# A skipped turn ahead of TensorE's loop, logits two tiles back, and other orders of group work and loads

## The reference

```python
ret = (scale * q @ k.T * Dmat) @ v          # per batch and head; Dmat: causal powers of gamma
x = ret of all heads side by side            # 4608 x 512
logits = x @ phi                             # 4608 x 32
d = softmax of logits over tokens;  c = softmax of logits over slots
slot_in = d.T @ x                            # 32 x 512
slot_out = relu(slot_in[e] @ w1[e]) @ w2[e]  # expert by expert, 4 slots each
y = c @ slot_out
out = ((y @ f1) * (y @ f2)) @ w3 @ w_out     # 4608 x 512
```

## Time and profile before

| | |
|---|---|
| time, median of 3 runs | 393.9 us (393.32 to 394.62) |
| profiled execution, its own time | 393.96 us |
| its span | 392.2 us |
| TensorE busy | 354.2 us (90% of the span) |
| DVE, ACT, POOL busy | 165.3, 125.7, 161.8 us |
[...]
| moved by DMA | 104.77 MB, mean 267 GB/s |

### The profile page before, as it was taken

How to read it: one execution, slowest core, us unless ns; L and a number is a source line. 1 busy time by engine, 2 the same in 40 slices (tenths; PEclk the granted TensorE clock), 3 DMA queues, 4 the chain that set the end, 5 groups by cost and what they waited for, 6 DMA issues and landing times. The chain is left out here.

```text
span 392.2 us, 16043 instructions
## 1 busy us (share of the span) xinstructions
PE 354.2 (90%) x7123; PEld 272.9 (70%) x7123; DVE 165.3 (42%) x329; ACT 125.7 (32%) x276; POOL 161.8 (41%) x155
## 2 busy tenths in 40 slices
PE   1557787899999999899999999899999999999996
PEld 1446676778878878664656555478878888888885
DVE  0333444557657656573013000699853323233320
ACT  1001112322423332222324220532734444434442
POOL 1621222323334542033546451298955554554530
PEclk9988989999999999999999999999999999999999
DMA  7995999768878887879999996058226655556322
GB/s 246 422 370 208 391 427 427 282 241 300 300 246 297 311 308 229 306 288 418 424 428 424 427 425 277 3 90 236 75 92 235 225 188 191 191 176 234 116 107 107
DMA packets 25914, 104.77 MB, mean 267 GB/s; under 512 B 2660, under 2 KB 5284, under 8 KB 16164
## 3 DMA queue, kind: packets, MB, share of 16 engines
q1 hardware_dynamic: 25892, 104.47, 71.2%
HBM read 94.14 MB, written 10.32 MB: 266 GB/s over the span
## 5 line engine op out<-in xcount | busy, mean ns | idle before, releaser
L558 POOL TENSOR_TENSOR pkg_sb<-pkg_sb,const_sb 128x512 f32<-128x512 f32 x36 | 37.5, 1042 | 106.9 <-DMA pkg_sb<-in_tiles 106.9
L620 POOL TENSOR_TENSOR feat<-c_sb 128x512 f32<-128x512 f32 x45 | 56.8, 1273 | 46.2 <-PE psum L988 44.3
L988 PE MATMUL psum<-m_hi,feat_hi 128*128 128x512 f32 x144 | 56.1, 390 | 0.3 <-DVE m_lo L1474 0.3
L988 PE MATMUL psum<-m_lo,feat_hi 128*128 128x512 f32 x144 | 56.0, 389 | 0.0
L988 PE MATMUL psum<-m_hi,feat_lo 128*128 128x512 f32 x144 | 56.0, 389 | 0.0
L427 DVE TENSOR_TENSOR feat_lo<-feat,feat_hi 128x512 fp32r<-128x512 f32 x34 | 27.2, 799 | 62.2 <-ACT feat_hi L1144 61.0
L1004 ACT COPY x_nat<-psum 128x512 f32<-128x512 f32 x36 | 21.1, 585 | 84.0 <-PE psum L700 84.0
L645 PE MATMUL psum<-pkg_sb 64*64 64x64 f32 x1152 | 26.4, 229 | 22.8 <-POOL pkg_sb L558 16.4
L1244 DVE TENSOR_TENSOR x_t<-psum,x_decay 128x512 f32<-128x512 f32 x36 | 24.9, 691 | 47.9 <-PE psum L690 47.9
L1144 ACT CAST feat_hi<-feat 128x512 fp32r<-128x512 f32 x45 | 28.1, 626 | 39.1 <-POOL feat L620 39.1
L690 PE MATMUL psum<-weights_t,pkg_sb 64*64 64x64 f32 x1152 | 32.4, 227 | 7.0 <-issue 4.9
(11 more groups left out here) (138 smaller groups left out, 569.3 us busy)
## 6 DMA issues: line engine op xcount, KB each, us to landing
pkg_sb<-in_tiles SPq DMA_DIRECT2D x34, 1024.0 KB, 4.8
unit_a<-in_units SPq DMA_DIRECT2D x16, 1024.0 KB, 14.5
c_sb<-c_rows SPq DMA_DIRECT2D x45, 256.0 KB
unit_x<-in_units SPq DMA_DIRECT2D x9, 1024.0 KB, 14.1
out<-out_sb SPq DMA_DIRECT2D x36, 256.0 KB, 2.0
fold_raw<-in_fold SPq DMA_DIRECT2D x6, 1024.0 KB, 11.6
unit_y<-in_units SPq DMA_DIRECT2D x5, 1024.0 KB, 12.2
unit_n<-in_units SPq DMA_DIRECT2D x4, 1024.0 KB, 11.6
```

What stands on the lines that cost most here:

```text
L558: nc.gpsimd.tensor_tensor(v_nat(n).rearrange("p (h d) -> p h d", h=HEADS), v_nat(n).rearrange("p (h d) -> p h d", h=HEADS), decay.unsqueez ...
L620: nc.gpsimd.tensor_tensor(feat[:, k, :], c_sb[:, s, x, :], c_sb[:, s, y, :], ALU.mult).then_inc(feat_ready, 1)
L988: last = mm(psum[:, OUT + b, :], x, y, start=(at == 0 and m == 0), stop=(at == 4 and m == 2))
```

## The change

TensorE's loop gets a tenth turn in front, i = 0. In it, each of the four steps is stepped over by a branch, and the scores and update of tile 0 (`first_steps`) run at the end of this turn, behind the steps in the code. In every other turn each step stands behind the same test, and the number of the turn in all other tests is one higher. Within a step, the order becomes: scores and update of the next tile, dispatch (one tile later than before), logits of the tile *two* before, the wait for `x_t` of the tile before, `through_states`, the wait for the copy of the logits, phase 0, `turn_x` of the tile before, phase 1. ACT copies logits before x accordingly and does group work one tile later; DVE does each part of the group work one tile later and ahead of `scale_x`. SP loads the constants first, and of the first two tiles the second half (k and v) ahead of the first (q and k turned); one unit follows tile 3 instead of two, two follow tile 4, two tile 5, one tile 8; the raw weights follow tiles 10, 11, 14 and 15. Behind the loop, the last logits stand ahead of the last `turn_x`.

The diff, cut to what the argument speaks of:

```diff
--- before.py
+++ after.py
@@ -53,6 +53,7 @@
 NAT_RING = 12
 QUARTERS = 4
 EARLY = 3
+FOLD_AT = (10, 11, 14, 15)
 FOLD_HI_AT, FOLD_LO_AT = (18, 22, 26), (21, 23, 25, 27, 29, 31)
 
 
@@ -458,11 +459,10 @@
                 sp.dma_start(pkg_sb[:, t, lo:hi], pkg[t].rearrange("(p c) -> p c", p=P)[:, lo:hi]
                              ).then_inc(tile_loaded[t] if half else first_loaded[t], 16)
 
-            load_first(0, 0)
             sp.dma_start(const_sb[:, 0:C_LATE], consts[:, 0:C_LATE]).then_inc(const_loaded, 16)
-            load_first(0, 1)
-            load_first(1, 0)
-            load_first(1, 1)
+            for t in range(2):
+                load_first(t, 1)
+                load_first(t, 0)
             sp.dma_start(x_decay[:, :, 0:P], consts[:, C_XDECAY:C_ALL].rearrange("p (a n) -> p a n", a=PAIRS)
                          ).then_inc(decay_loaded, 16)
             sp.dma_start(const_sb[:, C_LATE:C_XDECAY], consts[:, C_LATE:C_XDECAY]).then_inc(const_late_loaded, 16)
@@ -470,13 +470,16 @@
             load_tile(2)
             load_tile(3)
             load_first_unit(0)
-            load_first_unit(1)
             for n in range(SLOTS_IN, NTILES):
                 load_tile(n)
-                if n < 2 * SLOTS_IN:
-                    load_first_unit(n - 2)
-                elif n < 3 * SLOTS_IN:
-                    load_fold(n // 2 % 2 * 2, n % 2)
+                if n < SLOTS_IN + 2:
+                    load_first_unit(2 * n - 7)
+                    load_first_unit(2 * n - 6)
+                elif n == 8:
+                    load_first_unit(5)
+                elif n in FOLD_AT:
+                    at = FOLD_AT.index(n)
+                    load_fold(at // 2 * 2, at % 2)
 
             def load_unit(u):
 
...
@@ -694,12 +697,12 @@
                             last.then_inc(phase_done if phase == 0 else out_ready, 1)
                         elif phase == 1:
                             last.then_inc(phase_done, -1)
+                        elif half == 0:
+                            last.then_inc(x_t_ready if a == 0 else logits_copied, -1)
 
             def turn_x(r):
                 for a in range(PAIRS):
                     last = nc.tensor.transpose(psum[:, X_NAT, P * a:P * (a + 1)], x_t[:, r % 2, a, :], ident)
-                    if a < 2:
-                        last.then_inc(x_t_ready if a == 0 else logits_copied, -1)
                 last.then_inc(x_turned, 1)
 
             def logits(r):
@@ -714,7 +717,7 @@
             def dispatch(g):
 
                 pe.wait_ge(exp_nat_ready, g + 1)
-                pe.wait_ge(x_nat_ready, NTILES if g == GROUPS - 1 else dispatched_at(g))
+                pe.wait_ge(x_nat_ready, NTILES if g == GROUPS - 1 else dispatched_at(g) - 1)
                 def nat(t):
                     return x_nat[:, (g * TILES + t) % NAT_RING, :]
 
@@ -735,48 +738,51 @@
                 scores(r)
                 update(r)
 
-            def turn(r):
-
-                pe.wait_ge(logits_copied, 1)
-                pe.wait_ge(x_t_ready, 1)
-                turn_x(r)
-
             def step(i, r):
-                before, after = (r + SLOTS_IN - 1) % SLOTS_IN, (r + 1) % SLOTS_IN
+                two_before, before, after = [(r + m) % SLOTS_IN for m in (SLOTS_IN - 2, SLOTS_IN - 1, 1)]
 
                 if r < SLOTS_IN - 1:
                     next_scores(after)
                 else:
-                    with pe.If(i < NTILES // SLOTS_IN - 1):
+                    with pe.If(i < NTILES // SLOTS_IN):
                         next_scores(after)
-                if r > 0:
-                    turn(before)
+                for g in range(GROUPS - 1):
+                    if dispatched_at(g) % SLOTS_IN == r:
+                        with pe.If(i == dispatched_at(g) // SLOTS_IN + 1):
+                            dispatch(g)
+                if r > 1:
+                    logits(two_before)
                 else:
-                    with pe.If(i > 0):
-                        turn(before)
+                    with pe.If(i > 1):
+                        logits(two_before)
+
+                pe.wait_ge(x_t_ready, 1)
                 through_states(r)
+                pe.wait_ge(logits_copied, 1)
                 through_scores(r, 0)
                 if r > 0:
-                    logits(before)
+                    turn_x(before)
                 else:
-                    with pe.If(i > 0):
-                        logits(before)
-                for g in range(GROUPS - 1):
-                    if dispatched_at(g) % SLOTS_IN == r:
-                        with pe.If(i == dispatched_at(g) // SLOTS_IN):
-                            dispatch(g)
-
+                    with pe.If(i > 1):
+                        turn_x(before)
                 pe.wait_ge(phase_done, QUARTERS)
                 through_scores(r, 1)
 
-            pe.wait_ge(first_loaded[0], 16)
-            pe.wait_ge(v_ready, 1)
-            scores(0)
-            update(0)
-            pe.wait_ge(states_ready, 1)
-            with pe.Fori(0, NTILES // SLOTS_IN) as i:
+            def first_steps():
+
+                pe.wait_ge(first_loaded[0], 16)
+                pe.wait_ge(v_ready, 1)
+                scores(0)
+                update(0)
+                pe.wait_ge(first_loaded[1], 16)
+                pe.wait_ge(states_ready, 1)
+
+            with pe.Fori(0, NTILES // SLOTS_IN + 1) as i:
                 for r in range(SLOTS_IN):
-                    step(i, r)
+                    with pe.If(i > 0):
+                        step(i, r)
+                with pe.If(i == 0):
+                    first_steps()
 
             def fold_part(n):
 
@@ -852,9 +858,12 @@
                     if n is not None:
                         fold_part(n)
 
+            logits(SLOTS_IN - 2)
             fold(1)
-            turn(SLOTS_IN - 1)
+            pe.wait_ge(logits_copied, 1)
+            pe.wait_ge(x_t_ready, 1)
             logits(SLOTS_IN - 1)
+            turn_x(SLOTS_IN - 1)
             fold(5)
 
             dispatch(GROUPS - 1)
...
@@ -1080,27 +1090,28 @@
-            act.sem_inc(logits_copied, 1)
+            act.sem_inc(logits_copied, 2)
...
+                if g > 0 and n == dispatched_at(g - 1):
+                    copy_sums(g - 1)
+                if n > 1:
+                    copy_logits(n - 2)
+                copy_x(n - 1)
+                if g > 0 and t == 1:
                     move_parts(g - 1)
...
@@ -1300,6 +1311,7 @@
                 tt(c_nat[:, g * TILES:(g + 1) * TILES, :], comb[:, :, :],
                    comb_red[:, 3, 0:TILES].unsqueeze(2).to_broadcast([P, TILES, SLOTS]), ALU.mult).then_inc(c_ready, 1)
 
+            dve.sem_inc(x_t_ready, 1)
             dve.wait_ge(const_loaded, 16)
             nc.vector.memset(state_sb[:, 0, :, :].rearrange("p a n -> p (a n)"), 0.0)
             mask_scores(0)
@@ -1314,12 +1326,12 @@
                 else:
 
                     dve.sem_inc(states_ready, 1)
-                scale_x(n)
                 if g > 0:
-                    for at, part in ((0, max_parts), (1, max_slots), (2, turn_exp), (3, turn_raw), (4, max_combine),
-                                     (5, shift_combine), (6, sum_combine), (7, divide_combine)):
+                    for at, part in ((1, max_parts), (2, max_slots), (3, turn_exp), (4, turn_raw), (5, max_combine),
+                                     (6, shift_combine), (7, sum_combine), (8, divide_combine)):
                         if t == at:
                             part(g - 1)
+                scale_x(n)
 
             def w_low(half):
                 for f in range(4):
```

More of the change, by code:

```diff
@@ L380, in dispatched_at @@
         def dispatched_at(g):
-            return g * TILES + TILES + 3
+            return g * TILES + TILES + 4
         def chunks(engine, step):
@@ L490, in _ @@
                 if u == 9:
-                    sp.wait_ge(logits_ready, SUBS * NTILES)
+                    sp.wait_ge(x_turned, NTILES)
                 if u == 11:
@@ L1012, in copy_logits @@
                     act.wait_ge(exp_ready, g - 1)
-                copy(logits_raw[:, g % 2, SLOTS * t:SLOTS * (t + 1)], psum[:, RAW, 0:SLOTS]).then_inc(logits_copied, 1)
-                if t == TILES - 1:
+                copy(logits_raw[:, g % 2, SLOTS * t:SLOTS * (t + 1)], psum[:, RAW, 0:SLOTS]
+                     ).then_inc(group_copied if n == NTILES - 1 else logits_copied, 1)
+                if t == TILES - 1 and n < NTILES - 1:
                     copy(mark[:, :], const_sb[0:1, 0:1]).then_inc(group_copied, 1)
@@ L1081, in relu_hidden @@
                                          ACT.Relu).then_inc(hid_ready, 1)
-            act.sem_inc(logits_copied, 1)
-            for n in range(NTILES):
+            act.sem_inc(logits_copied, 2)
+            for n in range(1, NTILES):
                 g, t = divmod(n, TILES)
-                if n > 0:
-                    copy_x(n - 1)
-                    if g > 0 and n == dispatched_at(g - 1):
```

(14 more changed lines are left out.)

## The result

The changed kernel takes 399.28 us (median of 4 runs, 398.44 to 401.85) against 394.12 us: 1.4% slower, ratio 1.014 (95% interval 1.0102 to 1.0177). The forecast was 387.8 us, 382.0 to 392.5. The profiled execution took 399.35 us, its span is 397.6 us.

A forecast was written before the change was run, and what follows sets the result against it. Bytes were taken to bound the tile stage from 37 to 74 us, TensorE from then on. The sum was 394.0 - 22.2 + S + 1.5 = 373.3 + S, so 387.8 us with S = 14.5; range 382.0 to 392.5.

The forecast's parts named there:

- The start, S: Start of tile 0's scores, behind three code fetches in a row: 14.5 us, bounds 10.9 to 18.7; before 8.77.
- The hidden fetches: Rival for the turn in front: blocks arrive before transfers fill up, S 7.8 us, time 381.1 us; chance 0.13.
- TensorE starts too late: Rival: a fourth fetch or longer ones; S 19.8 or 24.6, time 393.1 or 397.9 us, slower; chance 0.09.
- 373.3: Forecast total in us without the start: 394.0 - 22.2 + 1.5; S is added to it.
- From S to tile 12: Bytes moved in SP's new order: tile 12 in at S + 49.1, its scores at S + 50.3, gain 22.2 - S.
- The hole: Idle transfers in the tile stage: earlier holes before 37 us close, a new one runs from some 18 us to S + 9.2.
- The bytes moved behind tile 12: Two of four raw blocks leave the queue ahead of tile 12: 4.9 us; sharing with tiles 14 and 15 costs at most 0.5.
- the full part: Tile stage from 37 to 74 us, taken as bound by bytes: DMA engines 0.98 busy at 401 GB/s.
- the stretch that has room: Where the two raw blocks go, behind tile 12; from 74 us TensorE was taken as the bound.
- The later turns: Loop turns of four tiles, 13.89 us before: +0.14 a turn; +1.5 us for all later effects, bounds -1 and +5.
- The new wait: Phase 0 waits for the logits' copy, ready at 0.91 us, TensorE there at 0.85: 0.06 a step, 0.24 a turn.
- the old three: Three dispatch tests a turn, ahead of phase 1 before: hidden behind the update, saving 0.42 us a turn.

The follow-up runs named there:

- experiment 6: Changed kernel with two branches in the turn in front, each over two steps, instead of four over one each: 400.71 us, ratio 1.0173.
- experiment 5: Changed kernel with SP holding the loads of tiles 2 and 3 and the unit behind them until tile 0's scores are done: 398.73 us, ratio 1.0136.
- experiment 15: Kernel before, with TensorE waiting ahead of tile 0's scores until tile 3 has landed, nothing else: 398.87 us, ratio 1.0115.
- Experiment 9: Changed kernel, turn in front kept, with all six first units behind tile 3: 393.96 us, ratio 1.0004.
- 10: Changed kernel without the turn in front, with all six first units behind tile 3: 394.76 us, ratio 1.0044.
- experiment 1: Changed kernel without the turn in front, all its other edits kept: 393.01 us, ratio 0.9992.
- experiment 3: Changed kernel with the units and raw weights placed as in the kernel before: 398.11 us, ratio 1.0108.
- 11: Changed kernel without the turn in front and with units and raw weights placed as in the kernel before: 393.38 us, ratio 0.9996.
- 13: Changed kernel without the turn; two units behind tile 3, raw weights quartered behind tiles 4 to 20, other units behind 15, 24, 33, 34: 390.28 us, ratio 0.9894.
- 14: Changed kernel with the turn; two units behind tile 3, raw weights quartered behind tiles 4 to 20, other units behind 15, 24, 33, 34: 392.98 us, ratio 0.9981.
- experiment 4: Kernel before with the new order of units and raw weights alone: 393.12 us, ratio 0.9993.
- experiment 2: Kernel before with the turn in front alone: 400.98 us, ratio 1.0194.

## Why the prediction was wrong

**The start, S: mis-sized.** The mechanism was there, and so were its parts: three jumps, one behind the other, the code behind them loaded and kept, no stall afterwards. In after the branches over the four steps (L782) begin at 1.0, 1.4, 6.7 and 12.1 us and last 0.36, 5.17, 5.35 and 7.25 us, and the q8 row counts one block from 19 to 30 us and none from 30 to 165. That this row is TensorE's code shows in the kernel before: its blocks begin to move at 16.1, 20.6, 26.4, 31.6 and 34.7 us (windows of 0.1 us), and TensorE resumes 2.2 to 2.7 us behind each (18.56, 22.80, 28.65, 34.06 and 37.38). Between two resumptions the trace has 204 to 233 matmuls and weight loads; the rest of the about 256 instructions, waits, branches and skipped code, is my count.

The size was off. I took 3.3 us for the first fetch and 4.7 for the others, S = 14.5, with 18.7 as the most I allowed. No run shows 3.3, 4.7 or 5.9 us as the time of a fetch: they are times between two resumptions, and that a fetch takes as long was my estimate. The runs show in their place what a jump took. Tile 0 started at 19.64: 6.2 us a jump over the 18.6 us from the first branch at 1.0 us. Two jumps took 11.9 us (experiment 6), 6.0 each, and three with the bulk loads held back 18.3 (experiment 5), 6.1 each. Five blocks were fetched by 19 us for three jumps, so two that nobody needed yet were in the row. Why a jump takes longer than the time between two resumptions, no run shows.

What I named as the reason for a long fetch, full transfers, holds in part. Where they ran out, a block moved 2.6 us (experiment 5) and 2.7 us (experiment 15) sooner behind the event before it. But experiment 5 took only 0.4 us off the start, so it is not what made S 5.1 us too small. The hidden fetches (0.13) are refuted: the third block moved at 9.6 us, beside full transfers (0.99 busy from 4.2 to 9.6 us).

The rival that came true is *TensorE starts too late*, given 0.09, and it named blocks in the row that no jump needed yet. Its edge was put at S = 20.7 us, which was not reached; the next two terms, as measured, move the edge to 14.3 us (394.1 less the 379.8 us that 373.3 becomes with them).

**From S to tile 12: the step that failed.** By my sum tile 12 would be scaled at S + 49.1 = 68.7; it was 73.94, another 5.2 us. Tile 8 was still on time (scaled at S + 33.2, its bytes in by S + 33.8 in the sum). Tile 9 was not: S + 40.1 instead of S + 36.3. The sum let its load wait for no slot. In the trace the slot comes free only at the end of a step that begins when tile 6 has landed, and the load went out at 55.01 us, S + 35.4; in front of tile 9 the transfers fell to 202 GB/s (55 to 58 us). Two things made it so late. 1.4 us are in the first step: tile 4's load went out at S + 8.6, not S + 7.2, as tile 1 starts 4.26 us behind tile 0 instead of 3.35 (the jump back to the loop's head now lies between them) and phase 1 follows later. And I held the step times at full clock. After TensorE had waited 3.85 and 2.68 us for tiles, its granted clock was 0.50 in the stretches behind both waits, and from 49.10 us to the load at 55.01 it took 5.9 us; the same stretch of a step at full clock takes 3.7 (58.31 to 62.00).

The hole itself was in the sum: it runs from the first loads to S + 9.2, and each microsecond of a later start makes it one longer. With S as measured it was 12 us long. Experiment 9 fills it and wins 5.3 us, where the same loads without the turn win nothing (10); experiment 15 makes one without a turn and loses 4.6.

**What the stalls cost where they stood.** The five stalls of the kernel before sum to 10.2 us. They were not free. The first fell ahead of tile 4's load and held it back until 19.41 us, while the first loads still moved (0.97 busy from 19 to 20 us); the others fell behind that load, and with them came the hole from 30 to 37 us. Where they stay in and the start is later, the late start is passed on whole (6.4 us at tile 12 in experiment 6 against 1); in experiment 15 the start is 8.6 us later, the first stall 2.9 us shorter, and tile 12 6.5 us later (77.89 us). After starts another 6.7 us later than experiment 6, without the stalls, and scales tile 12 1.9 us sooner. From these rows I estimate the loaded code at 8.6 us by tile 12 (6.7 + 1.9); the start it was bought with is 13.1 us later than in experiment 1 (19.64 less 6.56). No run takes the stalls away and leaves the start alone, so this stays an estimate. What the turn costs depends on what the transfers can do meanwhile: 6.3 us with the loads of after, 4.7 with those of before (3 against 11), 2.7 with those of 13 and 14, nothing with all units in the hole (9 against 10).

**The bytes moved behind tile 12: mis-sized.** Two raw blocks left the full part, as said; of the 4.9 us that this was to give, 3.1 came without the turn (experiment 4: tile 12 at 68.3 instead of 71.4) and none with it (73.94 against 73.90 in experiment 3). I allowed 0.5 us for tiles 14 and 15, with which they share. From tile 12 to 17 after takes 21.3 us (73.94 to 95.21), before 18.7; experiment 4 gives back 2.7 of its 3.1 us there. That they went "into the stretch that has room" was true of the mean (0.74 busy) and wrong of a single tile, which has only about 6.5 us from its issue to its scores (two steps of 3.47 less the 0.4 us by which the issue comes behind the step's end).

**The later turns: right.** +0.14 us a turn was forecast, +0.14 measured. The new wait is there as well: phase 0 starts 0.92 us behind the first load of the logits (97.48 to 98.40 us), 0.91 was forecast. The tests are 0.14 us each where nothing hides them (experiment 2), and the new order within the step hides the old three and the `x_t` wait: from tile 17 to 35 before takes 66.2 us, before with the turn 68.6, after 66.3, after without the turn 65.3. So the order within the step, which alone can't be told from none, saves 2.3 us where the turn is there.

Together: 5.1 us in S, 5.2 in the step to tile 12, 1.3 in what comes behind it (1.5 us were in the sum for it, 2.8 came) make the 11.6 us between forecast and profiled execution.

A jump's 6 us are mostly not the block's own move: in after the third block moves from 9.6 to 10.6 us, the fourth begins at 15.3, and in the 4.7 us between nothing of the code moves. In experiment 5, with idle transfers, that gap is 2.1 us. What happens in it stays open.

## What to carry to other kernels

Before a wait is moved, count what it costs at its new place, and ask what can be in flight there: ahead of the first release of a buffer, once the first loads are in, nothing is, unless loads that need no freed buffer are put there. Here a start 11 us later took away 10 us of stalls and lost 5 us. Skipping code to have it loaded cost some 6 us a jump in a row (6.0 to 6.2); it pays only if the engine would have had to wait that long for its first data anyway, or if other loads fill the time. Where the transfers are idle on the mean, a large load may still cost a tile its slack (0.74 busy from 74 to 95 us in the kernel before, and tiles 12 to 17 took 2.6 us more with raw weights behind 14 and 15); place it beside a step that is longer anyway.

## What was not expected of the hardware

In after the third block of code (16 KB) moved from 9.6 to 10.6 us, and the fourth began at 15.3, 4.7 us behind its end; the transfers were at 1.03 from 10.6 to 15.2 us, and TensorE stood at a branch from 12.1 us on, for 7.25 us (L782). In experiment 5 the third block ended at 12.5 us and the fourth began 2.1 us behind it, with the transfers at 0.00 from 12.5 to 14.6 us; the branch that began at 13.9 us took 4.99 us (L783). And the waits of after that end at 41.73 and 49.10 us, 3.85 and 2.68 us long, were followed by a granted clock of 0.50 (rows below), while experiment 2, whose waits for tiles from 41 to 72 us were of 0.81 to 2.10 us, stayed at 1.00 from 37 to 74 us. In the first steps of after, from 19.64 us, the weight loads take 0.98 us for 32, as long as those at 0.50, although the row for 18 to 30 us gives 1.00. Busy times of the kernel after in the stretches before and behind the waits that end at 41.73 and 49.10 us (the third number from the end is the granted clock), and in front of tile 9:

```profile
31.00:37.50 6.50, 6.50 (x328) 5.79 (x324) 4.09 (x8) 1.48 (x4) 2.05 (x2) 1.00 1.01 429
...
41.80:44.80 3.00, 3.00 (x116) 2.82 (x120) 1.12 (x2) 0.18 (x1) 0.00 (x0) 0.50 1.01 426
...
49.20:53.50 4.30, 4.30 (x146) 4.00 (x147) 1.54 (x3) 0.18 (x1) 1.69 (x2) 0.50 1.01 427
...
55.00:58.00 3.00, 3.00 (x148) 2.65 (x140) 2.14 (x4) 0.18 (x1) 0.00 (x0) 0.93 0.60 202
```
